# Two sizes of expert tile, the first layer's weights rounded in halves, and a second buffer for a load at the start

## What is computed

```python
# stage 1: a recurrence over 768 steps, for 4 batches x 8 heads of width 40
for t in range(S):
    y[:, :, t] = np.einsum('bhd,bhde->bhe', rt, state)
    Sa = np.einsum('bhde,bhe->bhd', state, at)
    state = state * wt[:, :, None, :] - np.einsum('bhd,bhe->bhde', Sa, bt) + np.einsum('bhd,bhe->bhde', vt, kt)
# stage 2: 3072 tokens of width 320, 8 experts of hidden width 1024, the two best of each token
top2 = np.argpartition(-noisy_logits, 2, axis=1)[:, :2]
for e in range(E):
    for k in range(2):
        mask = top2[:, k] == e
        h = np.maximum(x[mask] @ w1[e], 0.0)
        out[mask] += top2_w[mask, k, None] * (h @ w2[e])
# stage 3: a dense pair of layers, 320 -> 2048 -> 320
h = x @ w_in
out = np.maximum(0.01 * h, h) @ w_out
```

## Time and profile before

| what | value |
|---|---|
| median of three runs | 1472.08 us |
| the profiled execution | 1466.51 us, span 1464.7 us |
| TensorE busy | 1279.5 us, 87% of the span |
| VectorE busy | 949.2 us, 65% |
| ScalarE busy | 655.8 us, 45% |
| GpSimd busy | 300.7 us, 21% |
| moved by DMA | 197.71 MB, 135 GB/s on average |

### The profile page before, as it was taken

How to read it: one execution, slowest core, us unless ns; L and a number is a source line. 1 busy time by engine, 2 the same in 40 slices (tenths; PEclk the granted TensorE clock), 3 DMA queues, 4 the chain that set the end, 5 groups by cost and what they waited for, 6 DMA issues and landing times. The chain is left out here.

```text
span 1464.7 us, 39369 instructions
## 1 busy us (share of the span) xinstructions
PE 1279.5 (87%) x16046; PEld 1166.8 (80%) x16046; DVE 949.2 (65%) x1619; ACT 655.8 (45%) x1453; POOL 300.7 (21%) x262
## 2 busy tenths in 40 slices
PE   4468797878888974999999999999939999999998
PEld 3347586756776764999999999999938888988987
DVE  8969676885938008678878788888734445455343
ACT  3325353433443321566766677666613332333332
POOL 1116262532623221111111111111033022020000
PEclk9989898878989885899999999999979999999999
DMA  7563635536233302687776776778621011010000
GB/s 232 142 166 94 170 115 142 152 112 163 90 102 104 101 29 66 209 266 230 235 259 223 258 244 221 266 229 245 198 60 57 19 37 54 1 54 18 0 19 18
DMA packets 158694, 197.71 MB, mean 135 GB/s; under 512 B 62725, under 2 KB 117229, under 8 KB 158573
## 3 DMA queue, kind: packets, MB, share of 16 engines
q1 hardware_dynamic: 133492, 147.96, 33.4%
q10 hardware_dynamic: 19801, 29.94, 6.6%
q0 software_dynamic: 5280, 18.03, 4.3%
HBM read 171.57 MB, written 24.31 MB: 134 GB/s over the span
## 5 line engine op out<-in xcount | busy, mean ns | idle before, releaser
L349 DVE TENSOR_TENSOR prod<-Tl,Lt 128x1 f32<-128x1 f32 (+30 forms) x186 | 154.1, 829 | 54.6 <-DMA Lt<-lscr 48.5
L1296 DVE TENSOR_TENSOR gf<-psM,low 128x512 f32<-128x512 f32 x96 | 66.3, 691 | 177.8 <-ACT low L1334 177.8
L1334 ACT ACTIVATE low<-psM 128x512 f32<-128x512 f32 x96 | 57.5, 599 | 241.1 <-PE psM L1392 241.1
L1002 PE MATMUL psE<-w2h,hh 128*128 128x320 f32 x496 | 155.8, 314 | 0.0
L1004 PE MATMUL psE<-w2h,hl 128*128 128x320 f32 x496 | 153.3, 309 | 0.0
L1003 PE MATMUL psE<-w2l,hh 128*128 128x320 f32 x496 | 153.3, 309 | 0.0
L1089 POOL DMA_INDIRECT xs<-xrow,src x62 | 60.9, 982 | 410.3 <-PE psE L971 371.7
L987 PE MATMUL psE<-xh,w1h 128*128 128x256 f32 x496 | 141.5, 285 | 1.9 <-DVE xh L836 1.9
L988 PE MATMUL psE<-xl,w1h 128*128 128x256 f32 x496 | 141.4, 285 | 0.0
L989 PE MATMUL psE<-xh,w1l 128*128 128x256 f32 x496 | 141.4, 285 | 0.0
L836 DVE TENSOR_TENSOR w2l<-w2t,w2h 128x320 fp32r<-128x320 f32 x248 | 122.0, 492 | 16.2 <-ACT w2h L831 16.2
(11 more groups left out here) (185 smaller groups left out, 3104.0 us busy)
## 6 DMA issues: line engine op xcount, KB each, us to landing
w2t<-in_w_dram SPq DMA_DIRECT2D x31, 1280.0 KB, 6.7
w1t<-in_w_dram SPq DMA_DIRECT2D x31, 1024.0 KB, 8.7
w1t<-in_w_dram SPq DMA_DIRECT2D x62, 256.0 KB, 9.3
Vd<-in_vG_dram ACTq DMA_DIRECT2D x44, 320.0 KB, 4.5
ysort<-ys SPq DMA_DIRECT2D x31, 320.0 KB, 4.6
RV<-in_rvE_dram ACTq DMA_DIRECT2D x44, 208.0 KB
P<-in_wR_dram SPq DMA_DIRECT2D x24, 209.6 KB
U<-in_wE_dram SPq DMA_DIRECT2D x24, 209.6 KB
```

The costliest lines, as they stand in the source:

```text
L349: mark(nc.vector.tensor_tensor(prod[:, 0:t, 0:t], Tl[:, 0:t, CH - t:CH], Lt[:, t:t + 1, CH - t:CH].to_broadcast([128, t, t]), ALU.mult))
L1002: mm(o, hh[:, f, sl], w2h[:, f, :], start=(f == 0), stop=False)
```

## The change

- `TS` stays 256, but the sorted order has 55 blocks of 128 places: 23 tiles of 256 ("pairs") and `NSG` = 9 tiles of 128 ("singles"), 32 tiles, 7040 places. An expert with an odd number of blocks gets one single.
- The loop runs over four tiles: pair, single, pair, pair. The last four are pair, single, single, pair.
- In a single, the first layer's matmuls move 128 columns, the second layer has 3 matmuls for each `f` in place of 6, there are 3 transposes, and `hh`, `hl`, `xh`, `xl` are half as wide. The weights are loaded and split in full for every tile.
- The next tile's first weights are split in two halves of the hidden width: the first after `f == 3`, beside the first layer, the second after the rows. The split of the second weights runs two blocks behind: `w2h` and `w2l` of block `f-2` come after `hh` and `hl` of block `f`. ScalarE's wait for `w2t` stands at `f == 2`.
- Routing: three more operations of 192 elements on VectorE and some of 8 before the places are known; the computation of `texp` is moved behind the first half of the one-hot rows (`experts()`).
- Stage A: the suffix of group 1 is loaded into `U[:, 2]`, without a wait; group 2's goes into `P`, earlier; `decays(2)` comes later, after `to_blocks(0)`; `xT` is zeroed on GpSimd.

```diff
-NTS = (2 * TOK + E * (TS - 1)) // TS
+NBK = (2 * TOK + E * 127) // 128
+NSG = 9
+NPR = (NBK - NSG) // 2
+NTS = NPR + NSG
@@ stage_a, SyncE
-            for h in range(4):
-                sp.dma_start(P[:, 4 * h:4 * h + 4, :], wR[0][:, 4 * h:4 * h + 4, :]).then_inc(q[f"l_p{h}"], 16)
+            suffix_in(0)
             decays(0)
             wide_a(0)
             wide_b(0)
             wide_k(0)
+            suffix_in(1)
             decays(1)
-            suffix_in(1)
             out_half(0, 0)
             out_half(0, 1)
             to_lanes(0)
             wide_k(1)
             chunk(0)
             chunk(1)
-            decays(2)
+            suffix_in(2)
...
             to_blocks(0)
-            suffix_in(2)
+            suffix_free(2)
+            decays(2)
@@ stage_a, GpSimd and VectorE
+            nc.gpsimd.memset(xT[:, :, :, :], 0.0).then_inc(q["z_g"], 1)
-            nc.vector.memset(xT[:, :, :, :], 0.0).then_inc(q["z_v"], 1)
-            dve.wait_ge(q["z_v"], 4)
+            dve.wait_ge(q["z_v"], 3)
@@ stage_re, ScalarE
-                act.wait_ge(q["e_ld2"], i * 16 + 16)
                 for f in range(NF):
-                    split_hi(nc, w2h[:, f, :], w2t[:, f, :]).then_inc(q["e_w2h"], 1)
                     act.wait_ge(q["e_mm1"], i * NF + f + 1)
-                    nc.scalar.activation(hh[:, f, :], ps[2 + f % 4][:, 0:TS], ACT.Relu).then_inc(q["e_hh"], 1)
+                    nc.scalar.activation(hh[:, f, 0:W], ps[2 + f % 4][:, 0:W], ACT.Relu).then_inc(q["e_hh"], 1)
+                    if f == 2:
+                        act.wait_ge(q["e_ld2"], i * 16 + 16)
+                    if f >= 2:
+                        second_w(f - 2)
+                    if f == 3 and not final:
+                        act.wait_ge(ld[1 - p], (n + p) * LD + LD)
+                        first_w(1 - p, 0)
+                second_w(6)
+                second_w(7)
                 if not final:
-                    act.wait_ge(ld[1 - p], (n + p) * LD + LD)
-                    rows_and_w1(i + 1, 1 - p, n + p)
+                    rows(i + 1, TS if ahead[0] else 128)
+                    first_w(1 - p, 1)
@@ stage_re, VectorE
                 for f in range(NF):
-                    dve.wait_ge(q["e_w2h"], i * NF + f + 1)
-                    split_lo(nc, w2l[:, f, :], w2t[:, f, :], w2h[:, f, :]).then_inc(q["e_w2l"], 1)
                     dve.wait_ge(q["e_hh"], i * NF + f + 1)
...
+                    if f >= 2:
+                        second_w(i, f - 2)
+                    if f == 3 and not final:
+                        first_w(i + 1, 1 - p, 0)
+                second_w(i, 6)
+                second_w(i, 7)
                 if not final:
-                    rows(i + 1, 1 - p)
-                    first_w(i + 1, 1 - p)
+                    rows(i + 1, TS if ahead[0] else 128)
+                    first_w(i + 1, 1 - p, 1)
@@ stage_re, VectorE, routing
             for j in range(2):
+                if j:
+                    experts()
                 for f in (slice(0, 12), slice(12, 24)):
```

More of the change, by code:

```diff
@@ new lines, in slot, with seen @@
+        def slot(u, c, tail=False):
+            pair, at = place(u, c, tail)
+            back = (place(u - 1, c + 2, False) if c < 2 else place(u, c - 2, tail))
+            ahead = place(u, c + 1, tail) if c < 3 else place(u + 1, 0, False)
+            return u * 4 + c, c % 2, u * 2 + c // 2, pair, at, back, ahead
+        def seen(u, c, pair):
+            if not pair:
+                return 16 * (u + 1) if c == 1 else 16
+            return {0: u * 64 + 32, 2: u * 64 + 64, 3: u * 32 + 32}[c]
@@ L954, in _ @@
             tiles(sp, tile)
[L955 removed]
+            for c in (2, 3):
+                i, p, n, pair, at, back, ahead = slot(NU - 1, c, True)
                 sp.wait_ge(q["e_yA"], i + 1)
                 sp.wait_ge(q["e_yV"], i + 1)
[L958 removed]
+                store(pair, at, p)
             sp.wait_ge(wr[0], 16 * (NTS - NTS // 2))
@@ L999, in tile @@
                     pe.wait_ge(q["e_w2l"], i * NF + f + 1)
-                    for s in range(NS):
+                    for s in range(NS if pair else 1):
                         o, sl = ps[6 + s][:, 0:DM], slice(s * 128, s * 128 + 128)
@@ L1031, in tile, with first_w, second_w @@
+            def first_w(p, z):
+                half = slice(z * F1 // 2, z * F1 // 2 + F1 // 2)
+                split_hi(nc, w1h[:, :, half], w1t[:, p, :, half]).then_inc(q["e_w1h"], 1)
+            def second_w(f):
+                split_hi(nc, w2h[:, f, :], w2t[:, f, :]).then_inc(q["e_w2h"], 1)
+            def tile(u, c, first, final, tail):
+                i, p, n, pair, at, back, ahead = slot(u, c, tail)
+                W = TS if pair else 128
                 if first and p == 0:
                     act.wait_ge(ld[0], LD)
-                    for j in range(3):
-                        split_hi(nc, w1h[:, j, :], w1t[:, 0, j, :]).then_inc(q["e_w1h"], 1)
+                    first_w(0, 0)
+                    first_w(0, 1)
@@ L1081, in _ @@
             pool.wait_ge(q["r_src0"], 1)
+            where = {b: t for t, b in enumerate(list(range(4)) + [2 * NPR] + list(range(4, 2 * NPR)) + list(range(2 * NPR + 1, NBK)))}
             for i in range(NTS):
-                if i == NH0 // NS:
+                pair, at = place(i // 4, i % 4, i // 4 == NU - 1)
+                if i == 3:
                     pool.wait_ge(q["r_src"], 1)
@@ L1115, in tile, with second_w @@
+            def second_w(i, f):
+                dve.wait_ge(q["e_w2h"], i * NF + f + 1)
+                split_lo(nc, w2l[:, f, :], w2t[:, f, :], w2h[:, f, :]).then_inc(q["e_w2l"], 1)
+            def tile(u, c, first, final, tail):
+                i, p, n, pair, at, back, ahead = slot(u, c, tail)
+                W = TS if pair else 128
                 if first and p == 0:
-                    rows(0, 0)
+                    rows(0, TS)
                 for f in range(NF):
-                    dve.wait_ge(q["e_w2h"], i * NF + f + 1)
```

212 lines of the change are left out of this document (137 added, 75 removed).

## The result

| | before | changed |
|---|---|---|
| median | 1472.34 us (4 runs, 1465.31 to 1474.95) | 1583.30 us (4 runs, 1578.10 to 1587.22) |
| the profiled execution | 1466.51 us, span 1464.7 | 1584.51 us, span 1582.7 |

The changed kernel is slower: the ratio is 1.0746, with a 95% interval of 1.0716 to 1.0776, some 110 us. The forecast was 1456 us in a range of 1441 to 1475. It is wrong in its sign, and the time lies 108 us above the range.

The account below looks back on a forecast made before the run. TensorE's stream was taken to bound the expert stage, a third of the time. Stage A -5.5, routing +3.7, experts -10.8 gave -12.6: 1453.9 from the profiled 1466.5, set at 1456 us towards the higher median; range 1441 to 1475.

Parts of the forecast that it names:

- Expert stage, a pair: Expert stage, tile of 256 places: splits in the new order stay hidden behind TensorE, so a tile takes 15.35 us.
- Rival 1: Expert stage: the load of `w2t` becomes the bound from 7.3 us on; +17 us in the stage, 1482 us; chance 0.13.
- Rival 2: Expert stage: few columns cost more per matmul, a single takes 17.5 us, stage +34, 1499 us; chance 0.06.
- Rival 3: Expert stage: a single takes as long as a pair less 0.5 us; stage 0 to -2, 1464 to 1472; chance 0.11.
- Rival 4: Expert stage: cheap columns and short loads, a single at 11 us, stage -20, 1444 us; chance 0.14.
- A single's matmul: Expert stage, first layer: a matmul of 128 columns costs 0.115 us, taken between 0.07 and 0.12.
- A single: Expert stage, tile of 128 places: 11.9 us, bound by VectorE, plus 0.3 lost to the late load of `w2t`.
- The stage: Expert stage as a whole: 465.1 us against 475.9, -10.8, with bounds of -18 and -8.
- Routing: Between stage A and the expert stage: extra operations and a later `texp` delay the transposes by 3.7 us (2.5 to 6).
- Stage A: Stage A: group 1's scans start earlier without waiting for `P`, saving 5.5 us (between 3 and 6.5).
- The sum: Whole kernel: stage A -5.5, routing +3.7 and expert stage -10.8 give -12.6 us.

Follow-up runs that it names:

- experiment 1: Changed kernel with one edit: SyncE loads the next tile's first weights a tile ahead, before the store and the wait for `w2t`'s load; 1462.26 us, 0.9944 of before.
- experiment 6: Changed kernel, either with both halves of the first weights after the rows (1467.23 us) or with only that early half kept, second weights' splits in old order (1550.41 us).
- experiment 2: Kernel before, with its 31 tiles, routing and stage A, given only the new order of the splits; 1556.42 us, 1.0609 of before.
- experiment 7: Changed kernel, new split order kept, with the first weights loaded a tile ahead and the second weights loaded in two halves; 1457.19 us, 0.9896 of before.
- experiment 3: Changed kernel with the old order of the splits; new tile sizes, routing and stage A stay; 1457.42 us, 0.9916 of before.
- experiment 5: Changed kernel with the old order of the splits and the second weights loaded in two halves; 1451.86 us, 0.9847 of before.
- experiment 4: Kernel before with only the changed stage A; 1462.34 us, 0.9954 of before.
- experiment 8: Changed kernel, old split order, stage A chunk loads moved: first, ScalarE issues them later, `w2t` in halves (1469.70 us); second, SyncE issues them, `w2t` whole (1473.26 us).

## Why the prediction was wrong

**The step that failed** is *Expert stage, a pair*. It puts "the half until 6.05" behind `w2h(1)`, as if `w1t` lay ready. It had costed the load of `w2t` with its issue, its landing and its user, and for `w1t`, in the same queue on SyncE, it named neither. The rows of before held all that was needed. `w1t` is issued 1.3 us behind `w2t`; by that part's own numbers, with `w2l(7)` at T + 11.65 and a tile of 15.35, that is 2.4 us before the next T. It lands 9.1 us later, at T + 6.7. The half wants it at T + 4.65 (6.05 less its own 1.4). The step would have found it some 2 us late, then seen that lateness moves `w2l(7)`, that `w2l(7)` holds SyncE, and that SyncE holds the next `w1t`. By the prediction's own figures the loop is 1.3 + 9.1 + (11.65 - 4.65) = 17.4 us, an estimate, and already longer than TensorE's 15.35. A delay inside a loop isn't paid once: the period becomes the loop's sum, measured at 18.7, with 10.3 from the issue of `w1t` to its use. Experiment 1 shows the load's place to be the cause, experiment 6 that the early half is what needs the load early, experiment 2 that the loss is there without the sizes.

**Rival 1** had the right form and the wrong load. It asked from which landing time `w2t` decides (7.3 us), and the loads stayed at 6.3. With `w1t` out of the way it became real and small: 12 us in the stage (experiments 1 and 7). **Rival 2** is ruled out: 128 columns cost 0.111, fewer columns don't cost more. **Rival 3**, that the change doesn't shorten a single, is ruled out as well: a single costs 11.95 in experiment 3, a pair 15.37. **Rival 4** wanted a single at 11 and 20 us off the stage; a single stayed near 12.

**Point by point, where the loop is undone:**
- *A pair*: 15.35 predicted. With its loads ahead (experiment 7) a pair that follows a pair takes 15.1 to 15.3, so the rest of that step held.
- *A single's matmul*: 0.115 predicted, taken between two rows; 0.111 in the changed kernel and in experiment 3. The Trainium skill ("TensorE: Matmul & The Clock Gate", Back-to-back issue gap), with its 81 ns for a pair at 128 columns, doesn't hold for this type; the measurement decides.
- *A single*: 11.9 with VectorE as its bound, TensorE waiting 0.7 at its end, and 0.3 for `w2t`. In the new order with both loads ahead (experiment 7) it is 12.1 from start to start, with a wait of 0.38 for VectorE, and 11.8 net in the cycle (57.94 - 46.1). In the old order (experiment 3) it is 12.2, with a wait of 0.73, and 11.95 net. The load's part was nothing in the old order (experiment 5). In the new one it was 12 us in the stage, where the prediction had 9 x 0.3 = 2.7: mis-sized. Of the 12, the pair behind the first single lost 2.1, the second single and the pair behind it 1.5 each, each later cycle about 0.7, and the two neighbouring singles at the end 1.2 and 2.3.
- *The stage*: -10.8 predicted, as 465.1 against 475.9. Both leave out the stage's start, which the measured lengths hold, so only the differences can be compared. Before is 478.9 by that measure; experiment 3 has 463.9 (-15.0), experiment 1 473.6 (-5.3), experiment 7 461.6 (-17.3). The term was 4.2 us (experiment 3) to 6.5 us (experiment 7) too small for a stage with its loads in time. The last of the 9 singles, put at 14.4, is about half of that: nine singles and 23 pairs at the cycle's prices (11.95 and 15.37) give -15.4.
- *Routing*: +3.7 predicted, `texp` at 574.6. Measured `texp` at 574.17, the first gather at 587.57 (586.8 predicted); from routing's start to the first expert matmul 49.3 us against 45.8, +3.5. The second batch, which answers to the earlier trace rows, ends where the transposes begin, so that path decides:

```profile
582.99 10.43 PE L1070 MATMUL psE<-woh,wih 128*128 128x50 f32 x48 [1.65 <-DVE woh L1291]
593.25 1.54 PE L1021 MATMUL psE<-ident,xs 128*128 128x128 f32 x6
```

- *Stage A*: -5.5 predicted, -6.8 measured (experiment 4). The steps were right where they could be read: the scans run from 24.85 and last 4.60 as in the earlier trace rows, the prefix begins at 29.70. The inverse begins at 44.16, 3.9 earlier and not 5 to 6. The four products ahead of it take 5.7 us instead of 4.6, which stays unexplained, and `Lt` is waited for 0.82: its source was written at 26.84, as before (26.83), and not 1 to 2 us earlier, and it was read back from 38.24 instead of 37.74. By group 1's end the copy of the inverse is issued 6.5 us earlier than before (151.22 against 157.68), but routing begins only 0.3 earlier in the changed kernel, and where the gain goes stays open (experiments 4 and 8). The zeroing on GpSimd took 1.80 us and ended as the first scan began, so nothing here shows how the two engines disturb each other, and the Trainium skill's rule ("GPSIMD Engine Reference", Specifications) wasn't put to the test.
- *The sum*: -12.6. The kernel that has all the parts and not the loop, experiment 7, saves 15.3 us (10.2 to 20.4). That the sums are close is in part luck. In experiment 7's profiled execution, 10.5 us shorter than that of before, stage A gives -1.3 where -5.5 was forecast, routing +3.5 (+3.7), the expert stage -17.3 (-10.8), and what follows it is 4.6 us longer, where nothing was forecast and the cause is open. The term that was left out, the wait for `w1t`, was worth 117 us in the expert stage: 591.0 in the changed kernel against 473.6 with that load a tile ahead (experiment 1).

Every kernel without the loop but the second of experiment 8 is faster than before by an interval that leaves out 1. The fastest are experiment 5 (0.9847) and experiment 7 (0.9896).

## What to carry to other kernels

When work is moved to an earlier place, list everything that it reads, and for each load write down its issue, its landing and the new time of need. A load that was never waited for has no row among the waits, and so is easily left out. Then follow the issuing queue: if the load stands behind a wait for something that the moved work itself delays, the delay comes back around, and the period becomes the sum of that loop, here 18.7 us where the busiest engine needs 15.4. And of a gain in front of shared DMA queues a single trace shows one outcome; the runs of the part alone say what it is worth.

## What the runs showed of the hardware

- Load-and-matmul pairs of this type with 128 x 128 weights follow each other in 0.111 us with 128 columns (experiment 3) and 0.12 with 256 at full clock. At half clock it is 0.214 us with 50 columns (593.25 - 582.99 over 48) and 0.213 with 256 (the changed kernel, 597.03 to 599.80 over 13). Between 50 and 256 columns the number hardly counts.
- In the changed kernel the tile shown has its first layer at full clock. Then TensorE stands idle for 3.45 us before 764.14, for `w2l`, and the rest of the second layer runs at half clock (granted 0.66 from 761 to 767, 0.50 behind that). Two matmuls of 320 columns start 0.267 apart there, which is 320 / 1.2 GHz, against 0.147 in the tile before. Over the stage the granted clock is 0.90 instead of 0.99:

```profile
765.35 0.47 PE L1056 MATMUL psE<-w2l,hh 128*128 128x320 f32 x1
765.62 0.47 PE L1057 MATMUL psE<-w2h,hl 128*128 128x320 f32 x1
```

- A copy of 0.5 MB (`Tl`, 128 x 1024 of 4 bytes) issued 0.9 us behind another queue's loads took 6.9 us until the next transfer could be issued, instead of 2.75 when it was issued 4.8 us behind them.
